# Two slots instead of four for an expert's token numbers and gates, three weight chunks split earlier, and semaphores raised earlier in a routed MLP

## The chip, the cores and the metric

The kernel runs on one core of one Trainium2 chip. The metric is the device time of one execution in microseconds (us). Three runs of the kernel before gave 426.74, 427.00 and 428.26 us, the median being 427.0. Engines are named TensorE (PE, its weight loads PEld), VectorE (DVE), ScalarE (ACT), GpSimd (POOL) and SyncE (SP).

## The reference

Three stages follow one another, all in float32.

```python
# linear attention with decay, B, H, S, D = 2, 8, 768, 48
for t in range(S):
    cur = einsum('bhd,bhe->bhde', u * k[t], v[t])
    y[t] = einsum('bhd,bhde->bhe', r[t], state + cur)
    state = w * state + einsum('bhd,bhe->bhde', k[t], v[t])
# MLP on x = y as 1536 rows of 384, 2048 wide
h = x @ w_in
x = (max(h, 0) + alpha * min(h, 0)) @ w_out
# routed MLP: 8 experts, 1024 wide, each row to its best expert, capacity 384
expert = argmax(x @ w_gate, axis=1);  gate = softmax(x @ w_gate)[expert]
disp[expert, place in order of rows] = x
out[row] = gate[row] * (max(disp[e] @ w1[e], 0) @ w2[e])[place]
```

## The kernel before

**Numbers.** Each float32 product is made of three matmuls of a faster type. A value is split into a high part (a ScalarE copy) and a low part (value less high part, a subtraction on VectorE or GpSimd), and high x high, high x low and low x high are added in PSUM. So every weight chunk, every activation and every routed row passes through a "high" and a "low" operation. split_high and split_low do this for the chunks, named by their number c; the eight chunks of an expert follow one another, and chunks 16 to 31 belong to experts 0 and 1.

**Stages.** Attention runs to about 65 us, the first MLP in four groups of 384 rows to about 270 us, and the routed MLP to the end. While the first MLP makes its rows, they are scattered by indirect DMAs to a table in HBM, a stretch for each expert. The first 256 rows of expert 0 are worked early. After that the experts follow in turn: expert 0 written out by itself, then experts 1 to 7. A block of 384 rows (three tiles of 128) is loaded for each expert, and the counts of rows are read into registers, which choose the path at run time. With up to 128 rows an expert takes the short path: flip_up multiplies the 128 rows with the whole first weight matrix in two halves of 512 columns (L1702), VectorE applies the relu (flip_relu, L1215), TensorE turns the result (flip_turn, L1723), ScalarE and VectorE make its high and low parts (flip_high, L848, and flip_low, L1221), and flip_down multiplies it with the second matrix (L1652, L1667). Between the two halves of flip_turn the rows of the next expert are turned (turn_xe, L1570) and split (xe_high, L817, and xe_low, L1175). With more than 128 rows it is expert_up for eight chunks (L1601), each followed by relu (ScalarE, L793) and relu_low (VectorE, L1159), then expert_down for the second tile (L1632) and flip_down for the first. A third tile is added above 256 rows. In this data experts 0, 5, 6 and 7 go the short way, experts 1 to 3 the one for two tiles, and expert 4 has three. (Expert 0's count is after the early rows are taken off.)

**Weights of experts 2 to 7.** SyncE loads w1 and w2 pieces into w1_raw and w2_raw. In the turn of expert e, ScalarE and VectorE split w2 of expert e+1 (split_high2, L810, and split_low2, L1166). When e's own rows are through the first matrix (s_w1free), ScalarE splits w1 of expert e+2 (split_high1, L801, in w1_and_y), and GpSimd makes the low parts (split_low1, L636). Among the copies of w1_and_y stand the y_copy (L834) of expert e, which scale its rows by their gates; GpSimd scatters them to the output by their token numbers (y_scatter, L612).

**Token numbers and gates.** A loaded row carries its token number and its gate behind its 384 values. keep_meta(e) on VectorE (a cast, L1183, and a copy, L1184) takes them out of the loaded block xe, of which there are two, into the buffers token and gate, of which there are four. It runs at the end of VectorE's turn for expert e-1. It may overwrite a slot only when the scatters that read it have landed. For that it waits for s_gone, which starts at 1 and which GpSimd raises in its own turn for expert e (1 to 6), behind the eight split_low1 of expert e+2 and a wait for the scatters up to expert e-1:

```python
                if 0 < e < E - 1:
                    pool.wait_ge(s_out, e * 16 * GT)
                    pool.sem_inc(s_gone, 1)
                for i in Y_ORDER:
                    y_scatter(e, i, s_out if e < E - 1 else s_last)
```

**Order.** Nothing plans this at run time: each engine's instructions are written out in order, and semaphores bind the engines together. All that stands behind a wait in an engine's queue waits too. Around expert 0, ScalarE has split_high(29) and (30), flip_high(0, 0, first half), xe_high(1, 0), split_high(31), flip_high(0, 0, second half), xe_high(1, 1) and (1, 2), then w1_and_y(0). VectorE has the two flip_relu, flip_low, xe_low(1, 0), flip_low, xe_low(1, 1) and (1, 2), split_low(29) to (31) for the second matrix, and keep_meta(1). GpSimd makes the low parts of these chunks' first matrix itself (L508). SyncE's load_xe(e) waits for s_meta, the count of keep_meta done, to reach e-1.

Of the kernel before, what the change touches and what calls it, by code (L numbers as in the profile page):

```python
# [3 lines left out]
P = 128  # L4


def attention_moe_kernel(nc, att_rk, att_v, decay, bonus, chunks, alpha, w_gate, out, disp,
# [8 lines left out]
    f32, f32r, bf16, i32 = mybir.dt.float32, mybir.dt.float32r, mybir.dt.bfloat16, mybir.dt.int32  # L16
# [15 lines left out]
    GT = G // P  # L32
# [115 lines left out]
    slot_i = mlp.take("slot_i", [P, GT], i32)  # L148
    xe = mlp.take("xe", [P, 2, GT, ROW], f32)
    y_out = mlp.take("y_out", [P, 2, GT, DM], f32)  # L150
    token = mlp.take("token", [P, 4, GT], i32)
    gate = mlp.take("gate", [P, 4, GT], f32)
    early_token = mlp.take("early_token", [P, ET], i32)
    early_gate = mlp.take("early_gate", [P, ET], f32)
    late = Region(phase_from, LIMIT)
# [13 lines left out]
    with ctx:  # L169
# [311 lines left out]
        def _(pool):  # L481
# [127 lines left out]
            def y_scatter(e, i, done=s_out):  # L609

                pool.wait_ge(s_yo, e * GT + Y_ORDER.index(i) + 1 + C_YO)
                pool.indirect_dma_start(  # L612
                    out=out, out_offset=bass.IndirectOffsetOnAxis(ap=token[:, e % 4, i:i + 1], axis=0),
                    in_=y_out[:, e % 2, i, :], in_offset=None, bounds_check=N - 1,
                    oob_is_err=False).then_inc(done, 16)

# [35 lines left out]
        def _(act):  # L652
# [167 lines left out]
            def y_copy(e, i):  # L820

                act.wait_ge(s_yzero, 1)
                act.wait_ge(s_meta, e + 1)
                act.wait_ge(s_gone, max(e - 1, 0) + C_GONE)
                if e == 1:
                    act.wait_ge(s_outa, 16 * ET)

                if i:
                    act.wait_ge(s_yd[i], e + 1)
                    if 0 < e < E - 1:  # L830
                        act.wait_ge(s_tel, e * GT + GT - i + 1)
                else:
                    act.wait_ge(s_step, e * NFE + NFE + FFN_STEPS)
                act.activation(y_out[:, e % 2, i, :], bank[4 + i][:, 0:DM], ACT.Copy,  # L834
                               scale=gate[:, e % 4, i:i + 1]).then_inc(s_yo, 1)

            act.wait_ge(s_cnti, 2)
            rows = [rows_of(act, e) for e in range(E)]
# [24 lines left out]
            with act.Else():  # L863
# [3 lines left out]
                    flip_high(0, i)  # L867
                for i in range(1, GT):
                    y_copy(0, i)
            for c in range(2 * NF - 3, 2 * NF - 1):  # L870
                split_high(c)
            flip_high(0, 0, (0,))
            xe_high(1, 0, bank[X_BANK[0]])
            split_high(2 * NF - 1)
            flip_high(0, 0, (1,))
            for i in range(1, GT):
                xe_high(1, i, bank[X_BANK[i]])
# [33 lines left out]
        def _(dve):  # L911
# [266 lines left out]
            def keep_meta(e):  # L1178

                xe_there(dve, e, range(GT))  # L1180

                dve.wait_ge(s_gone, max(e - 3, 0) + C_GONE)
                dve.tensor_copy(token[:, e % 4, :], xe[:, e % 2, :, DM:DM + 1].rearrange("p a b -> p (a b)"))  # L1183
                dve.tensor_copy(gate[:, e % 4, :], xe[:, e % 2, :, DM + 1:ROW].rearrange("p a b -> p (a b)"))\  # L1184
                   .then_inc(s_meta, 1)

            early_low(4)
# [44 lines left out]
            with dve.Else():  # L1232
                for i in range(1, GT):
                    xe_low(0, i, bank[8 - i])
                for i in range(1, GT):
                    for half in range(2):
                        flip_relu(0, i, half)
                    for half in range(2):
                        flip_low(0, i, half)
            flip_relu(0, 0, 0)  # L1240
            flip_relu(0, 0, 1)
            flip_low(0, 0, 0)
            xe_low(1, 0, bank[X_BANK[0]])
            flip_low(0, 0, 1)
            for i in range(1, GT):
                xe_low(1, i, bank[X_BANK[i]])
            for c in range(2 * NF - 3, 2 * NF):
                split_low(c)
            keep_meta(1)

            for e in range(1, E):
# [39 lines left out]
        def _(pe):  # L1291
# [387 lines left out]
            def no_tile(i):  # L1679

                pe.sem_inc(s_yd[i], 1)
# [84 lines left out]
            def expert(e, b):  # L1766

                rows = rows_of(pe, e)
                with pe.If(rows < P + 1):
                    pe.wait_ge(s_tel, (e - 1) * GT + GT)  # L1770
                    pe.sem_inc(s_mh, NFE)
                    for half in range(2):
                        flip_up(e, 0, half, b)
                    flip_turn(e, 0, (0,))
                    if more(e):
                        for i in range(GT):
                            x_bank_free(e, i)
                            turn_xe(e + 1, i, bank[X_BANK[i]], 1 - b)
                    no_tile(1)
                    flip_turn(e, 0, (1,))  # L1780
                with pe.Else():
                    pe.wait_ge(s_tel, (e - 1) * GT + GT)
                    pe.sem_inc(s_fh[0], 2)
                    pe.sem_inc(s_ft[0], 2)
                    expert_ups(e, 2 * P, b)
                    expert_down(e, 1, b)
                with pe.If(rows < 2 * P + 1):
                    flip_down_high(e, 0, 0, b)
                    pe.sem_inc(s_w1free, 1)
                    pe.sem_inc(s_fh[2], 2)  # L1790
                    no_tile(2)
                    flip_down_low(e, 0, 0, b)
                    flip_down_high(e, 0, 1, b)
                    flip_down_low(e, 0, 1, b)
                    pe.sem_inc(s_ft[2], 2)
                with pe.Else():
                    for half in range(2):
                        flip_up(e, 2, half, b)
                    pe.sem_inc(s_w1free, 1)
                    expert_down(e, 0, b, range(HF))  # L1800
                    flip_turn(e, 2)
                    expert_down(e, 0, b, range(HF, NFE))
                    flip_down(e, 2, b)
# [71 lines left out]
```

## Time and profile before

| | |
|---|---|
| median of three runs | 427.0 us (426.74 to 428.26) |
| the profiled execution | 427.0 us, span 425.3 us |
| TensorE matmul busy | 404.7 us, 95% |
| VectorE busy | 259.7 us, 61% |
| GpSimd busy | 230.7 us, 54% |
| ScalarE busy | 192.2 us, 45% |
| TensorE's share of the chain that ended last | 68% |
| granted TensorE clock, mean | 0.997 |

The span runs from the first instruction to the last, and the execution's own time is 1.7 us longer. TensorE is busy for nearly all of it; the others have slack on average, but each of them can be the last to be ready at a given point. In a timeline row the first number is the start from the span's beginning, the second the duration, and a bracket at the end says how long the engine had been idle before and for whom it waited. Operations of one engine overlap a little at their ends in these rows.

### The profile page before, as it was taken

What the parts mean: (1) busy time and instruction counts of PE and PEld (TensorE: products, weight loads), DVE (VectorE), ACT (ScalarE), POOL (GpSimd) and SP (SyncE); (2) the same over time, 40 slices, a digit from 0 to 9 for tenths busy, and PEclk for the clock granted to TensorE, in tenths of its full rate; (3) what the DMA queues carried; (4) which work ended last, traced back from release to release, by engine and by line L of the source; (5) the groups of instructions that cost most, each with busy time, mean ns of one, the idle gap of its engine ahead of it and who ended that gap; (6) DMA issues with size and microseconds to landing.
All of it is one profiled execution on the core that took longest, in us unless ns stands there. A gap on an engine that the chain in (4) does not pass through costs nothing.

```text
span 425.3 us, 9352 instructions
## 1 busy us (share of the span) xinstructions
PE 404.7 (95%) x3194; PEld 387.6 (91%) x3195; DVE 259.7 (61%) x523; ACT 192.2 (45%) x442; POOL 230.7 (54%) x239
## 2 busy tenths in 40 slices
PE   5799999999999999999999999999999999999893
PEld 4688899999999999999999999998998989899682
DVE  6888877765436344263343888573977594735960
ACT  2879955441311113111132243345849577536851
POOL 3999818563322633236353586054949375528862
PEclk9999999999999999999999999999999999999998
DMA  7997027437970100001000256039976685817500
GB/s 242 403 364 242 3 73 215 142 93 260 370 254 2 37 19 0 0 0 37 19 0 0 74 173 191 28 98 327 311 259 197 207 234 187 270 35 225 178 11 28
DMA packets 34330, 61.74 MB, mean 145 GB/s; under 512 B 4798, under 2 KB 27310, under 8 KB 34288
## 3 DMA queue, kind: packets, MB, share of 16 engines
q1 hardware_dynamic: 31280, 55.92, 40.3%
q0 software_dynamic: 3008, 5.29, 3.6%
q8 instruction: 22, 0.36, 0.4%
q14 instruction: 20, 0.16, 0.1%
HBM read 47.92 MB, written 15.18 MB: 148 GB/s over the span
## 4 chain that ended last, share of the span: by engine, by line
PE 68%; DVE 11%; issue 6%; ACT 5%; PEld 5%; POOL 2%; PEldq 1%; DMA 0%; ACTq 0%; DVEq 0%; POOLq 0%
PE bank L1418 24%; PE bank L1379 23%; DVE w_low L1166 4%; PE bank L1702 3%; PE bank L1363 3%; ACT w_high L801 3%; PE bank L1327 2%; PEld bank L1632 2%; PE bank L1355 2%; DVE expert_g_low L1159 2%; PE bank L1519 2%; PE bank L1632 2%; PE bank L1652 1%; PE bank L1313 1%; DVE xe_low L1175 1%
## 5 line engine op out<-in xcount | busy, mean ns | idle before, releaser
L554 POOL TENSOR_TENSOR g_low<-act_full,g_high 128x384 fp32r<-128x384 f32 x63 | 65.2, 1035 | 111.2 <-ACT g_high L708 111.1
L708 ACT ACTIVATE g_high<-act_full 128x384 fp32r<-128x384 f32 x64 | 33.7, 526 | 146.8 <-DVE act_full L1041 134.2
L1379 PE MATMUL bank<-x_split,w_high 128*128 (+1 forms) x384 | 98.6, 337 | 0.2 <-DVE w_low L954 0.2
L1035 DVE TENSOR_SCALAR neg<-bank,alpha_sb 128x384 f32<-128x384 f32 x64 | 39.4, 616 | 89.2 <-PE bank L1379 89.2
L636 POOL TENSOR_TENSOR w_low<-w_raw,w_high 128x384 fp32r<-128x384 f32 x48 | 52.9, 1137 | 33.9 <-ACT w_high L801 33.9
L1379 PEld LDWEIGHTS bank<-x_split,w_high 128*128 128x128 f32 x384 | 68.9, 188 | 0.9 <-DVE w_low L954 0.5
L1418 PE MATMUL bank<-w_high,g_high 128*128 128x384 f32 x189 | 64.5, 341 | 0.0
L1379 PE MATMUL bank<-x_split,w_low 128*128 (+1 forms) x192 | 64.4, 336 | 0.0
L1418 PE MATMUL bank<-w_high,g_low 128*128 128x384 f32 x189 | 63.8, 338 | 0.0
L1418 PE MATMUL bank<-w_low,g_high 128*128 128x384 f32 x189 | 63.8, 338 | 0.0
L1041 DVE SCALAR_TENSOR_TENSOR act_full<-bank,neg 128x384 f32<-128x384 f32 x64 | 35.7, 557 | 2.4
L1166 DVE TENSOR_TENSOR w_low<-w_raw,w_high 128x384 fp32r<-128x384 f32 x48 | 36.4, 775 | 0.3 <-ACT w_high L810 0.3
L1418 PEld LDWEIGHTS bank<-w_high,g_high 128*128 128x128 f32 x189 | 35.4, 187 | 0.8 <-POOL g_low L554 0.7
L1379 PEld LDWEIGHTS bank<-x_split,w_low 128*128 128x128 f32 x192 | 36.0, 188 | 0.0
L1418 PEld LDWEIGHTS bank<-w_low,g_high 128*128 128x128 f32 x189 | 35.5, 188 | 0.0
L1418 PEld LDWEIGHTS bank<-w_high,g_low 128*128 128x128 f32 x189 | 35.4, 187 | 0.0
L954 DVE TENSOR_TENSOR w_low<-w_raw,w_high 128x384 fp32r<-128x384 f32 x44 | 32.0, 755 | 0.0
L612 POOL DMA_INDIRECT out<-y_out,token x24 | 25.0, 1043 | 10.8 <-issue 5.4
L679 ACT ACTIVATE scores<-ident,diag 128x128 f32<-128x128 f32 x96 | 29.3, 394 | 2.6 <-DVE diag L969 2.6
L1601 PE MATMUL bank<-xe_high,w_high 128*128 128x256 f32 x96 | 27.7, 289 | 0.0
L662 ACT ACTIVATE w_high<-w_raw 128x768 fp32r<-128x768 f32 x32 | 26.8, 836 | 1.2 <-DMA w_raw<-chunks 1.2
L1601 PE MATMUL bank<-xe_high,w_low 128*128 128x256 f32 x96 | 27.1, 282 | 0.0
(171 smaller groups left out, 847.5 us busy)
## 6 DMA issues: line engine op xcount, KB each, us to landing
w_raw<-chunks SPq DMA_DIRECT2D x96, 192.0 KB, 4.4
w_raw<-chunks SPq DMA_DIRECT2D x32, 384.0 KB, 3.7
rk_in<-att_rk SPq DMA_DIRECT2D x12, 704.0 KB, 6.1
routed_rows<-fill SPq DMA_DIRECT2D x1, 5211.0 KB, 18.0
xe<-routed_rows SPq DMA_DIRECT2D x7, 579.0 KB, 4.4
v_in<-att_v SPq DMA_DIRECT2D x12, 200.0 KB, 5.7
out<-fill SPq DMA_DIRECT2D x1, 2304.0 KB, 23.3
x_split<-x_split POOLq DMA_DIRECT2D x18, 48.0 KB, 2.7
```

Source lines behind the costliest of these rows:

```text
L554: pool.tensor_tensor(gl[:, f % 4, :], act_full[:, f % 2, :], gh[:, f % 4, :].bitcast(f32), ALU.subtract).then_inc(s_gl, 1)
L636: pool.tensor_tensor(wl[:, slot, 0:W1], raw1[:, f, :], wh[:, slot, 0:W1].bitcast(f32), ALU.subtract).then_inc(s_wl1e, 1)
L662: act.activation(wh[:, slot, :], raw[:, m, :], ACT.Copy).then_inc(s_wh, 1)
L679: last = act.activation(scores[:, t % 2, h % 2, h // 2, :], ident[:, :], ACT.Copy, scale=diag[:, t % 2, h:h + 1])
L708: act.activation(gh[:, f % 4, :], act_full[:, f % 2, :], ACT.Copy).then_inc(s_gh, 1)
L954: dve.tensor_tensor(wl[:, slot, part], raw[:, m, part], wh[:, slot, part].bitcast(f32), ALU.subtract).then_inc(s_wl1 if first else s_wl2, 1)
L1035: dve.tensor_scalar(neg[:, f % 2, :], h, 0.0, alpha_sb[:, f:f + 1], ALU.min, ALU.mult)\
L1041: dve.scalar_tensor_tensor(act_full[:, f % 2, :], h, 0.0, neg[:, f % 2, :], ALU.max, ALU.add)\
L1166: dve.tensor_tensor(wl[:, slot, W1:CW], raw2[:, f, :], wh[:, slot, W1:CW].bitcast(f32), ALU.subtract).then_inc(s_wl2, 1)
L1379: last = mm(bank[f % 4][:, 0:G], a[:, f, w], x[:, kc, bass.ds(g * G, G)], start=kc == 0 and i == 0, stop=kc == KC - 1 and i == 2)
L1418: last = mm(bank[4 + i][:, 0:DM], a[:, f % 4, i * P:(i + 1) * P], w[:, slot, W1:CW], start=f == 0 and m == 0, stop=f == n - 1 and m == 2)
L1601: last = mm(bank[f % 4][:, 0:n], a[:, slot, w], x[:, b, kc, 0:n], start=kc == 0 and i == 0, stop=kc == KC - 1 and i == 2)
```

## The change

Four edits are made together.

- token and gate have two slots, indexed by e % 2. keep_meta(e) waits for s_gone to reach max(e-1, 0) + 1 instead of max(e-3, 0) + 1.
- ScalarE splits chunk 31 right behind chunks 29 and 30, ahead of flip_high(0, 0, (0,)) and xe_high(1, 0).
- VectorE makes the low parts of chunks 29 to 31 between flip_relu(0, 0, 0) and flip_relu(0, 0, 1), not behind xe_low(1, 2).
- TensorE, in an expert of at most 256 rows, raises s_w1free, s_fh[2] and s_yd[2] before flip_down instead of after its first eight matmuls, and on the short path s_yd[1] after the second half of flip_turn instead of before it.

```diff
-    token = mlp.take("token", [P, 4, GT], i32)
-    gate = mlp.take("gate", [P, 4, GT], f32)
+    token = mlp.take("token", [P, 2, GT], i32)
+    gate = mlp.take("gate", [P, 2, GT], f32)
...
# y_scatter (GpSimd) and y_copy (ScalarE): e % 4 becomes e % 2
...
# ScalarE
-            for c in range(2 * NF - 3, 2 * NF - 1):
+            for c in range(2 * NF - 3, 2 * NF):
                 split_high(c)
             flip_high(0, 0, (0,))
             xe_high(1, 0, bank[X_BANK[0]])
-            split_high(2 * NF - 1)
             flip_high(0, 0, (1,))
...
# VectorE, keep_meta(e)
-                dve.wait_ge(s_gone, max(e - 3, 0) + C_GONE)
-                dve.tensor_copy(token[:, e % 4, :], xe[:, e % 2, :, DM:DM + 1].rearrange("p a b -> p (a b)"))
-                dve.tensor_copy(gate[:, e % 4, :], xe[:, e % 2, :, DM + 1:ROW].rearrange("p a b -> p (a b)"))\
+                dve.wait_ge(s_gone, max(e - 1, 0) + C_GONE)
+                dve.tensor_copy(token[:, e % 2, :], xe[:, e % 2, :, DM:DM + 1].rearrange("p a b -> p (a b)"))
+                dve.tensor_copy(gate[:, e % 2, :], xe[:, e % 2, :, DM + 1:ROW].rearrange("p a b -> p (a b)"))\
                    .then_inc(s_meta, 1)
...
# VectorE, expert 0
             flip_relu(0, 0, 0)
+            for c in range(2 * NF - 3, 2 * NF):
+                split_low(c)
             flip_relu(0, 0, 1)
             flip_low(0, 0, 0)
             xe_low(1, 0, bank[X_BANK[0]])
             flip_low(0, 0, 1)
             for i in range(1, GT):
                 xe_low(1, i, bank[X_BANK[i]])
-            for c in range(2 * NF - 3, 2 * NF):
-                split_low(c)
             keep_meta(1)
...
# TensorE, expert(e, b)
+                    flip_turn(e, 0, (1,))
                     no_tile(1)
-                    flip_turn(e, 0, (1,))
...
                 with pe.If(rows < 2 * P + 1):
-                    flip_down_high(e, 0, 0, b)
                     pe.sem_inc(s_w1free, 1)
                     pe.sem_inc(s_fh[2], 2)
                     no_tile(2)
-                    flip_down_low(e, 0, 0, b)
-                    flip_down_high(e, 0, 1, b)
-                    flip_down_low(e, 0, 1, b)
+                    flip_down(e, 0, b)
                     pe.sem_inc(s_ft[2], 2)
```

## Rows read from the trace of the kernel before

**Rows 1.** Busy time by stretch: PE, PEld, DVE, ACT, POOL, clock, DMA share, GB/s

```profile
300.00:330.00 30.00, 28.82 (x216) 28.36 (x215) 24.13 (x44) 22.17 (x55) 23.21 (x21) 1.00 0.77 248
```

**Rows 2.** Waits from 290 us: engine line, releaser: us in total, times, longest

```profile
PE bank L1632 <- DVE xe_low L1175: 2.9, 4, 0.9
```

**Rows 3.** Timeline of TensorE, experts 0, 1, 2 and 6

```profile
295.67 0.60 PE L1723 MATMUL bank<-ident,expert_g_by_token 128*128 128x128 f32 x4
...
310.37 0.44 PE L1632 MATMUL bank<-w_high,expert_g_high 128*128 128x384 f32 x1 [0.32 <-DVE xe_low L1175]
...
329.42 0.44 PE L1632 MATMUL bank<-w_high,expert_g_high 128*128 128x384 f32 x1 [0.86 <-DVE xe_low L1175]
...
402.89 0.66 PE L1723 MATMUL bank<-ident,expert_g_by_token 128*128 128x128 f32 x4 [1.73 <-DVE expert_g_by_token L1215]
```

**Rows 4.** Timeline of GpSimd, experts 0, 1 and 5

```profile
292.39 2.00 POOL L508 TENSOR_TENSOR w_low<-w_raw,w_high 128x384 fp32r<-128x384 f32 x2
...
317.47 8.54 POOL L636 TENSOR_TENSOR w_low<-w_raw,w_high 128x384 fp32r<-128x384 f32 x8 [5.12 <-ACT w_high L801]
...
394.89 9.49 POOL L636 TENSOR_TENSOR w_low<-w_raw,w_high 128x384 fp32r<-128x384 f32 x8 [2.16 <-ACT w_high L801]
```

**Rows 5.** Line L646: whole run, from 335, from 394 us; ns min/median/max, starts

```profile
L646 POOLq EVENT_SEMAPHORE  x6: 17/17/17, 321.3 to 409.8; - x6
...
L646 POOLq EVENT_SEMAPHORE  x1: 17/17/17, 340.3 to 340.3; - x1
...
L646 POOLq EVENT_SEMAPHORE  x1: 17/17/17, 398.7 to 398.7; - x1
```

**Rows 6.** Timeline of VectorE, end of expert 1 and start of expert 2

```profile
317.73 0.80 DVE L1183 CAST token<-xe 128x3 int32<-128x3 f32 x1
...
322.00 0.42 DVE L1159 SCALAR_TENSOR_TENSOR expert_g_low<-bank,expert_g_high 128x256 fp32r<-128x256 f32 x1 [3.40 <-ACT expert_g_high L793]
```

**Rows 7.** Lines L1183 (whole run) and L1166 (expert 2): ns min/median/max

```profile
L1183 DVE CAST token<-xe x8: 154/792/989, 289.9 to 408.4; 128x3 int32<-128x3 f32 x8
...
L1166 DVE TENSOR_TENSOR w_low<-w_raw,w_high x8: 542/544/1418, 322.4 to 331.3; 128x384 fp32r<-128x384 f32 x8
```

**Rows 8.** Timeline of VectorE, end of expert 5 and start of expert 6

```profile
397.62 0.99 DVE L1183 CAST token<-xe 128x3 int32<-128x3 f32 x1
...
398.60 0.68 DVE L1215 TENSOR_SCALAR expert_g_by_token<-bank 128x512 f32<-128x512 f32 x1
399.55 2.68 DVE L1166 TENSOR_TENSOR w_low<-w_raw,w_high 128x384 fp32r<-128x384 f32 x2 [0.28 <-ACT w_high L810]
402.16 0.68 DVE L1215 TENSOR_SCALAR expert_g_by_token<-bank 128x512 f32<-128x512 f32 x1
```

**Rows 9.** Timeline of VectorE, expert 0

```profile
292.40 0.69 DVE L1215 TENSOR_SCALAR expert_g_by_token<-bank 128x512 f32<-128x512 f32 x1 [2.30 <-PE bank L1702]
294.45 0.69 DVE L1215 TENSOR_SCALAR expert_g_by_token<-bank 128x512 f32<-128x512 f32 x1 [1.36 <-PE bank L1702]
...
298.81 3.66 DVE L954 TENSOR_TENSOR w_low<-w_raw,w_high 128x384 fp32r<-128x384 f32 x3
...
303.36 0.41 DVE L1159 SCALAR_TENSOR_TENSOR expert_g_low<-bank,expert_g_high 128x256 fp32r<-128x256 f32 x1
```

**Rows 10.** Line L388, chunks 30 and 31: issues, and us to landing

```profile
L388 SPq DMA_DIRECT2D w_raw<-chunks x2: 375/398/421, 287.2 to 287.8; - x2
...
DMA to landing us min/median/max: 5.1/5.9/6.7
```

**Rows 11.** Timeline of ScalarE, expert 0 and start of expert 1

```profile
292.32 0.85 ACT L662 ACTIVATE w_high<-w_raw 128x768 fp32r<-128x768 f32 x1 [0.98 <-DMA w_raw<-chunks]
...
295.83 0.85 ACT L662 ACTIVATE w_high<-w_raw 128x768 fp32r<-128x768 f32 x1
...
301.57 0.41 ACT L793 ACTIVATE expert_g_high<-bank 128x256 fp32r<-128x256 f32 x1
```

**Rows 12.** Line L1795, TensorE's queue: ns min/median/max, starts

```profile
L1795 PEldq EVENT_SEMAPHORE  x6: 51/51/51, 315.7 to 415.1; - x6
```

More of the change, by code:

```diff
@@ L612, in y_scatter @@
                 pool.indirect_dma_start(
-                    out=out, out_offset=bass.IndirectOffsetOnAxis(ap=token[:, e % 4, i:i + 1], axis=0),
+                    out=out, out_offset=bass.IndirectOffsetOnAxis(ap=token[:, e % 2, i:i + 1], axis=0),
                     in_=y_out[:, e % 2, i, :], in_offset=None, bounds_check=N - 1,
@@ L834, in y_copy @@
                 act.activation(y_out[:, e % 2, i, :], bank[4 + i][:, 0:DM], ACT.Copy,
-                               scale=gate[:, e % 4, i:i + 1]).then_inc(s_yo, 1)
+                               scale=gate[:, e % 2, i:i + 1]).then_inc(s_yo, 1)
             act.wait_ge(s_cnti, 2)
```

## The prediction

> **What bounds the kernel now.** I read the busy time by stretch first. TensorE is busy for 28.8 of the 30 us from 300 to 330, with the clock fully granted, while VectorE has 24.1 and GpSimd 23.2 [rows 1]. So the routed part, where every edit lies, is bound by TensorE with little idle, and an edit counts only by what it does to the few places where TensorE waits. The waits list says where these are: expert_down (L1632) waited 2.9 us in 4 times for xe_low on VectorE [rows 2]. The TensorE timeline gives them singly: 0.32 us in expert 1, 0.86 in expert 2, and 1.73 before the second gate-transposition (L1723) of expert 6 [rows 3]. Experts 1 to 4 take the path for over 128 rows, experts 0, 5, 6 and 7 the short one with flip_turn. Matmuls between the waits are packed, and whatever a wait adds is paid in full. VectorE, ScalarE and GpSimd run in chains that begin anew with each expert from TensorE's semaphores, so a delay of TensorE moves what follows and is not made up there.
>
> The profiled execution took 427.0 us, its span being 425.3 with 1.7 outside; the median of the three runs is 427.0 too, so changes of the span are added to 427.0 directly. About 0.5%, 2.1 us, is what a measurement of this kernel can tell from no change.
>
> **Part 1: keep_meta waits for two experts later.** token and gate go from four slots to two. That frees some SBUF and removes no instruction. The wait in keep_meta(e+1), on VectorE in expert e's turn, rises from s_gone at least e-1 to at least e+1. The (e+1)th count is added by GpSimd in its own iteration e (L646), behind the eight split_low1 of expert e+2 and a wait for the scatters of expert e-1. Behind the waiting VectorE stand relu_low(e+1, 0) (L1159) or flip_relu (L1215), and for these TensorE waits.
>
> When does the count come? GpSimd works at the eight subtractions from 317.47 to 326.01 [rows 4], but the increment at L646 stands in the trace at 321.3, in the next expert at 340.3 and in expert 5 at 398.7 [rows 5]. GpSimd's queue has thus handed over all eight when ScalarE has written the last w_high, and counts while the engine still works. So VectorE waits for ScalarE's last split_high1, not for GpSimd's work.
>
> In expert 1 keep_meta stands at 317.73 and the next relu_low at 322.00, which waited 3.40 us for ScalarE [rows 6]. Now the cast starts at about 321.35. Beside a busy GpSimd a cast takes 0.79 (the median of eight, 0.15 the least, 0.99 the most [rows 7]), and the next operation begins 0.8 to 0.98 after its start. That gives relu_low at 322.15 to 322.33, later by 0.15 to 0.33. In experts 1 to 3 that lands on the chain of VectorE which ends in TensorE's waits of some 0.86. I take 0.2, three times: **0.6 us** (0 to 1.0).
>
> Expert 4: the count comes late, since its w1_and_y waits for the third tile's y, but VectorE then has nothing before flip_relu(5), whose first half is needed by TensorE only after the second half of flip_up. I take nothing, at most 0.4. Expert 6: L646's last event is at 409.8 [rows 5], before flip_relu(7) would be due; nothing, at most 0.5.
>
> Expert 5 is dearer. keep_meta(6) starts at 397.62 and flip_relu(6, 0, 0) at 398.60, the subtractions (L1166) at 399.55, the second flip_relu follows, and TensorE waits for that one for 1.73 [rows 3, 8]. Now the cast starts at 398.75, flip_relu at 399.73 (+0.98), it ends at 400.35, and the subtractions begin 0.8 later than 399.55. All of it is in front of TensorE's wait: **0.8 us** (0.3 to 1.4, because the two subtractions, 2.68 us for both, run in turns with GpSimd's and may lose or win part of a turn).
>
> **Part 2: the last three chunks of expert 1 before flip_relu(0, 0, 1).** On ScalarE split_high(31) moves ahead of flip_high(0, 0, 0) and xe_high(1, 0); on VectorE three split_low (L954) move from behind xe_low(1, 2) to between the two flip_relu of expert 0. No instruction is added. Today the two flip_relu are at 292.40 and 294.45, and the three subtractions take 3.66 us from 298.81 [rows 9]. TensorE takes the second half's transposition at 295.67 without a wait [rows 3]. What sets the new time is chunk 31. The two load_chunk issues are at 287.2 and 287.8, and their landings take 5.1 and 6.7 us [rows 10]; as ScalarE stopped waiting for chunk 30 at 292.32 [rows 11], the 6.7 belongs to chunk 31: landed at 294.5. ScalarE copies it in 0.85 [rows 11], ready 295.3. VectorE has done the other two by then (from 293.09; GpSimd is at its own two until 294.39 [rows 4]). The third subtraction starts at 295.3, as does GpSimd's for the same chunk. One takes 0.54 us alone and up to 1.42 beside GpSimd [rows 7]; the three today average 1.22. I take 1.2 since both are released by one semaphore. So flip_relu(0, 0, 1) starts at 296.4, and TensorE 0.73 later (402.16 to 402.89 in expert 6 [rows 3, 8]), at 297.1 instead of 295.67: +1.4, between +0.8 (VectorE first) and +1.8.
>
> The Trainium skill, page "SBUF — State Buffer", on the ports of VectorE and GpSimd, says that a VectorE operation with two SBUF inputs and a GpSimd operation that reads SBUF take a shared port as an exclusive lock, the second being blocked until the first ends. By it the third subtraction has one of the two ends and not the mean; its order of issue decides, and the sum would be 0.6 us lower or 0.2 higher. The rows of 0.54 and 1.42 agree [rows 7].
>
> What comes back: VectorE is free of 3.66 us before expert 1. relu_low(1, 0) stands at 303.36 behind the subtractions and keep_meta(1), though ScalarE's relu was there at 301.57 [rows 9, 11]. With TensorE 1.4 later, relu(1, 0) ends about 303.3, so VectorE's chain stays where it is in time, and TensorE's wait of 0.32 at 310.37 is gone. ScalarE is 0.8 later with split_high1(2), which is still less than TensorE's delay. Net **1.1 us** (0.5 to 1.5). SP's order is untouched; its load_xe waits for s_meta, but behind load_w1 for GpSimd's work, which is later still.
>
> **Part 3: TensorE's own semaphores.** s_w1free, s_fh[2] and s_yd[2] are raised earlier by the eight matmuls of flip_down_high(e, 0, 0), and no_tile(1) after four transpositions instead of before. For experts 1 to 3 ScalarE's w1_and_y is held by flip_high(e, 2), which waits for s_ft[2] at L1795 (first event 315.7 [rows 12]), and that stays last. In experts 5 and 6 ScalarE comes to split_high1 later than w1free in any case. VectorE's flip_relu(e, 2), whose result nobody uses when the expert has no third tile, may start a little earlier and then waits for ScalarE as before. The order of matmuls is the same. Nothing, 0 to -0.3.
>
> **The sum:** 0.6 + 0.8 + 1.1 = 2.5 us, 427.0 + 2.5 = **429.5 us**. If this is right, the worst stall is still that before L1723 of expert 6, 2.5 us then.
>
> **Rivals.** (a) *The shifts are mostly absorbed.* The third subtraction goes first at the port (+0.5 net), the casts cost 0.14 each (0.4), and expert 5 wins part of a turn (0.3 to 0.4): 1.3 us, 428.3. The spread of the casts and of the subtractions speaks for it; against it, that before a busy GpSimd the long times are the common ones.
>
> (b) *Not slower: chunk 31 lands early.* It decides at L954: if the chunk lands in the 5.1 us of its neighbour, at 292.9, ScalarE has it by 294.0 and VectorE does three subtractions in a row from 293.09, ending near 295.2. TensorE then loses 0.1 to 0.5 and gets back 0.32 in expert 1. It holds up to a landing at about 293.5. With 0.4 to 0.8 of part 1 the time is 427.5. The transfers of eight w1 pieces are issued right behind and share the DMA engines, which speaks for 6.7 again.
>
> (c) *GpSimd counts only when its work is done.* Then keep_meta(2) would go at 326.0 [rows 4] and relu_low(2, 0) be 4.2 late; without GpSimd beside it VectorE wins back about 1.9 on three subtractions, leaving 2.3, three times 6.9. Expert 4 adds 1, expert 5 waits until 404.4 (394.89 and 9.49 [rows 4]) and costs 4 at the second flip_relu. With part 2, 13 us: 440. The events of L646 speak plainly against it.
>
> (d) *The port turns go worse*: 1.8 in part 2, 1.4 in expert 5, 0.33 per cast, 0.9 in experts 4 and 6: 5 us, 432.
>
> **How the numbers follow.** The forecast 0.46, (a) 0.25, (b) 0.12, (c) 0.07, (d) 0.10. The forecast's own span is 428.8 to 430.6. The range 427.4 to 432.6 holds all but (c) and the ends of the others. Slower by over 0.5% (above 429.1): five sixths of the forecast, (c) and (d), 0.56. Faster by over 0.5% (below 424.9) has no case that I can name: 0.02. The rest, 0.42, is within.
>
> **What would show it.** In the new profile: the cast of keep_meta at 321 to 323 and not 318, right behind L646's event, and relu_low(2, 0) 0.8 to 1.0 after it; no gap at L1632 of expert 1; a new gap of about 1.4 us before the second L1723 of expert 0; a gap of about 2.5 before that of expert 6; L646's events still some 4 us ahead of the end of GpSimd's eighth subtraction. It is wrong if the cast begins only when GpSimd is through, if TensorE has no gap in expert 0, or if a stall stands where I found none, in experts 4 and 6.

## The result

The changed kernel takes 430.78 us (median of 8 runs, 429.95 to 433.21) where the kernel before takes 427.04 (8 runs). The ratio is 1.0089 with a 95% interval of 1.0062 to 1.0115: 3.8 us slower (2.6 to 4.9), of which 2.5 had been forecast. The profiled execution, at 429.56 us and a span of 427.9, is the fastest of them, 2.6 us above that of before.

The profile of the changed kernel, busy time over the whole span (the kernel before has the same 9352 instructions):

```profile
span 427.9 us, 9352 instructions
PE 406.9 (95%) x3194; PEld 388.8 (91%) x3195; DVE 258.3 (60%) x523; ACT 192.6 (45%) x442; POOL 229.8 (54%) x239
```

The counts of instructions are the same for every engine. What moved is found in the timeline of TensorE, whose waits answer to [rows 3]. Of its rows with a gap, one of each kind is shown:

```profile
296.25 0.66 PE L1722 MATMUL bank<-ident,expert_g_by_token 128*128 128x128 f32 x4 [0.83 <-DVE expert_g_by_token L1214]
...
323.82 0.38 PE L1600 MATMUL bank<-xe_high,w_high 128*128 128x256 f32 x1 [0.18 <-DVE expert_g_low L1158]
329.88 0.44 PE L1631 MATMUL bank<-w_high,expert_g_high 128*128 128x384 f32 x1 [0.55 <-DVE xe_low L1174]
...
401.88 0.63 PE L1722 MATMUL bank<-ident,expert_g_by_token 128*128 128x128 f32 x4 [0.46 <-DVE expert_g_by_token L1214]
404.28 0.66 PE L1722 MATMUL bank<-ident,expert_g_by_token 128*128 128x128 f32 x4 [0.79 <-DVE expert_g_by_token L1214]
405.56 0.44 PE L1651 MATMUL bank<-w_high,expert_g_high 128*128 128x384 f32 x1 [0.62 <-DVE w_low L1165]
...
416.10 0.41 PE L1651 MATMUL bank<-w_high,expert_g_high 128*128 128x384 f32 x1 [0.53 <-issue]
```

There are four kinds of new gap: one before expert 0's second transposition (L1722), one in the middle of the first-matrix products of experts 2 to 4 (L1600), one before the first transposition of expert 6 (0.46), and one before the first matmul of flip_down (L1651) in experts 6 and 7. The old gap at L1631 of expert 1 is gone. The old wait of 1.73 before the second transposition of expert 6, which the prediction saw grow to 2.5, is 0.79. A list of gaps does not yet give what each edit cost, because a delay can hide in a later wait. For that I took each landmark's start less the start of flip_up of expert 0 in the same execution, and subtracted the same of the kernel before. The table gives this difference, the lag, in us, for the changed kernel and for the three edits made alone (below):

| landmark in TensorE's order | changed | slots alone | early split alone | semaphores alone |
|---|---|---|---|---|
| expert 0, second flip_turn | 0.99 | 0.00 | 1.88 | 0.00 |
| expert 1, expert_down | 0.46 | 0.00 | 1.35 | 0.21 |
| expert 2, expert_down | 0.87 | 0.44 | 1.34 | 0.18 |
| expert 3, expert_down | 1.34 | 0.91 | 2.31 | 0.23 |
| expert 4, expert_down | 1.82 | 1.36 | 2.31 | 0.27 |
| expert 5, second flip_turn | 1.81 | 1.36 | 2.29 | 0.25 |
| expert 5, flip_down | 2.24 | 1.36 | 2.29 | 0.69 |
| expert 6, second flip_turn | 1.80 | 1.64 | 2.52 | 0.29 |
| expert 6, flip_down | 2.43 | 1.64 | 2.52 | 0.92 |
| expert 7, flip_down | 2.99 | 1.65 | 4.04 | 1.45 |

(The changed kernel came to flip_up 0.41 us early, so that its span shows 2.6 and not 3.0.)

The end of VectorE's turn for expert 1 in the changed kernel, which answers to [rows 6]:

```profile
321.40 1.07 DVE L1182 CAST token<-xe 128x3 int32<-128x3 f32 x1 [3.56 <-POOLq L646]
322.39 1.06 DVE L1183 COPY gate<-xe 128x3 f32<-128x3 f32 x1
323.36 0.41 DVE L1158 SCALAR_TENSOR_TENSOR expert_g_low<-bank,expert_g_high 128x256 fp32r<-128x256 f32 x1
```

And GpSimd's work and its count at L646, which answer to [rows 4, 5]:

```profile
317.50 8.18 POOL L636 TENSOR_TENSOR w_low<-w_raw,w_high 128x384 fp32r<-128x384 f32 x8 [5.66 <-ACT w_high L801]
...
L646 POOLq EVENT_SEMAPHORE  x6: 17/17/17, 321.3 to 411.2; - x6
```

The cast starts 0.1 us after the count at 321.3, while GpSimd works until 325.7. So the count does run ahead of the engine. But the cast is held for 1.07 us and then the copy for 1.06 as well, where the copy had never cost more than 0.16 before. Each takes as long as one GpSimd subtraction (1.0) and ends with it.

### The profile page after: what moved, and what is told of

It reads as the page before. It is cut to its first block, busy times and chain, and to the rows that moved or that the text cites. A ratio compares the mean times of both kernels' runs of the same rounds, so it can differ in the third digit from the quotient of the medians.

```text
span 427.9 us, 9352 instructions
## 1 busy us (share of the span) xinstructions
PE 406.9 (95%) x3194; PEld 388.8 (91%) x3195; DVE 258.3 (60%) x523; ACT 192.6 (45%) x442; POOL 229.8 (54%) x239
## 4 chain that ended last, share of the span: by engine, by line
PE 69%; DVE 9%; issue 5%; PEld 5%; POOL 4%; DMA 3%; ACT 2%; SPq 0%; PEldq 0%; POOLq 0%; ACTq 0%; DVEq 0%
PE bank L1417 24%; PE bank L1378 23%; POOL w_low L636 4%; PE bank L1362 3%; PE bank L1701 3%; DVE w_low L1165 3%; PE bank L1326 3%; PE bank L1354 2%; PE bank L1651 2%; PE bank L1631 2%; PEld bank L1600 2%; PEld bank L1631 2%; DMA w_raw<-chunks 2%; PE bank L1312 1%; DVE expert_g_low L1158 1%
## 5 line engine op out<-in xcount | busy, mean ns | idle before, releaser
L636 POOL TENSOR_TENSOR w_low<-w_raw,w_high 128x384 fp32r<-128x384 f32 x48 | 50.8, 1090 | 37.8 <-ACT w_high L801 37.8
L1165 DVE TENSOR_TENSOR w_low<-w_raw,w_high 128x384 fp32r<-128x384 f32 x48 | 33.5, 714 | 0.0
L612 POOL DMA_INDIRECT out<-y_out,token x24 | 25.9, 1079 | 12.0 <-issue 5.5
L953 DVE TENSOR_TENSOR w_low<-w_raw,w_high 128x384 fp32r<-128x384 f32 x44 | 31.2, 736 | 0.2 <-ACT w_high L662 0.2
L1600 PE MATMUL bank<-xe_high,w_high 128*128 128x256 f32 x96 | 28.1, 293 | 0.7 <-DVE expert_g_low L1158 0.5
L1600 PE MATMUL bank<-xe_high,w_low 128*128 128x256 f32 x96 | 27.1, 282 | 0.0
```

Of the source, the lines that this page charges most:

```text
L636: pool.tensor_tensor(wl[:, slot, 0:W1], raw1[:, f, :], wh[:, slot, 0:W1].bitcast(f32), ALU.subtract).then_inc(s_wl1e, 1)
L953: dve.tensor_tensor(wl[:, slot, part], raw[:, m, part], wh[:, slot, part].bitcast(f32), ALU.subtract).then_inc(s_wl1 if first else s_wl2, 1)
L1165: dve.tensor_tensor(wl[:, slot, W1:CW], raw2[:, f, :], wh[:, slot, W1:CW].bitcast(f32), ALU.subtract).then_inc(s_wl2, 1)
L1600: last = mm(bank[f % 4][:, 0:n], a[:, slot, w], x[:, b, kc, 0:n], start=kc == 0 and i == 0, stop=kc == KC - 1 and i == 2)
```

## Each edit alone

All times below are against runs of the kernel before on the same chip. Its median went from 427.2 to 428.5 between these chips, so the ratios count, not the medians.

**The slots alone.** The kernel before with two slots (token and gate as [P, 2, GT], indexed by e % 2) and the wait of the change:

```diff
+                dve.wait_ge(s_gone, max(e - 1, 0) + C_GONE)
```

> The kernel before with two slots and the stronger wait of keep_meta alone. Theory 1 (from the changed kernel's trace): in experts 1 to 3 the cast starts 3.5 us later, with ScalarE's last split_high1, and then both small operations of keep_meta (1.07 and 1.06 us) wait for a GpSimd subtraction each; the first L1632 of experts 2, 3, 4 moves by 0.43 to 0.48 more each time, and in expert 5 the delay is made up again: span +1.3 us, time about 428.4. Theory 2 (the prediction's sizes): 0.2 each in experts 1 to 3 and 0.8 in expert 5, +1.4, so the same time but with the stall before the second L1723 of expert 6 longer than 2.3 us. Theory 3: the wait is nothing, 427.0.

Measured: 428.48 us, ratio 1.0023 (1.0009 to 1.0037), +1.0 us. Its trace has keep_meta as in the changed kernel:

```profile
321.17 1.07 DVE L1183 CAST token<-xe 128x3 int32<-128x3 f32 x1 [3.57 <-POOLq L646]
322.15 1.06 DVE L1184 COPY gate<-xe 128x3 f32<-128x3 f32 x1
323.12 0.41 DVE L1159 SCALAR_TENSOR_TENSOR expert_g_low<-bank,expert_g_high 128x256 fp32r<-128x256 f32 x1
```

The lag grows by 0.44, 0.47 and 0.45 in experts 1 to 3 and by 0.28 in expert 5. Theory 1 holds for the place, though in expert 5 the delay is not made up in full; the stall of over 2.3 us in expert 6 that theory 2 wanted isn't there.

**The early split alone.** ScalarE's and VectorE's part of the change's diff.

> The kernel before with chunks 29 to 31 split earlier on ScalarE and VectorE alone. Theory 1 (from the changed kernel's trace): about 1.0 us lost before the second transposition of expert 0, 0.55 won back in expert 1's first-matrix products and at its L1632: +0.45 us, about 427.5. Theory 2 (the prediction): +1.4 and 0.3 back, +1.1, 428.1. Theory 3: nothing is won back, because the wait of expert 1 comes from something else than VectorE's three subtractions: +1.0 with a wait of 0.3 still at L1632 of expert 1.

Measured: 428.23 us, ratio 1.0025 (1.0007 to 1.0043), +1.1 us. Its profiled execution, at 431.09 us, is the slowest of the twelve, so the trace shows where time can go and not what the edit costs as a rule. ScalarE's copies of chunks 30 and 31 in it, to be set against [rows 11]:

```profile
294.21 0.85 ACT L662 ACTIVATE w_high<-w_raw 128x768 fp32r<-128x768 f32 x1 [2.85 <-DMA w_raw<-chunks]
295.22 0.84 ACT L662 ACTIVATE w_high<-w_raw 128x768 fp32r<-128x768 f32 x1 [0.16 <-DMA w_raw<-chunks]
```

Chunk 31 was ready for its copy 5.1 us after flip_up's start at 290.09, against 4.5 in the changed kernel. Its transfer took as long in both (6.8 and 6.7 us), but was issued 0.6 later against flip_up. Chunk 30 was ready at 4.1 against 2.3, so that VectorE's second subtraction too had to wait. The third subtraction took 0.83 us, against 0.56. The second flip_turn of expert 0 was 1.88 late, in the changed kernel 0.99. Half a microsecond comes back both times in expert 1 (1.88 to 1.35, 0.99 to 0.46). So the price is set by when chunk 31 is there, and then by the turn of the third subtraction; both differ from one execution to the next. Two later jumps in this trace have nothing to do with the edit. The one in expert 3 is a single subtraction:

```profile
342.81 3.38 DVE L1165 TENSOR_TENSOR w_low<-w_raw,w_high 128x384 fp32r<-128x384 f32 x1
```

It ended only after three GpSimd operations in a row, and put TensorE back by 1.7 us, of which 0.8 were made up. The other, 1.6 us in flip_down of expert 6, is the clock. Busy time of PE, PEld, DVE, ACT and POOL, then the granted clock:

```profile
404.00:406.00 2.00, 0.56 (x4) 0.42 (x4) 2.00 (x4) 0.19 (x1) 2.00 (x3) 1.00 0.00 0
406.00:408.00 2.00, 2.00 (x7) 1.92 (x7) 2.00 (x5) 1.78 (x5) 1.85 (x2) 0.57 0.00 0
408.00:410.00 2.00, 2.00 (x8) 2.00 (x8) 2.00 (x6) 2.00 (x5) 1.39 (x3) 0.58 0.02 0
```

**The semaphores alone.** TensorE's part of the change's diff.

> The kernel before with only TensorE's semaphore increments moved. Theory 1 (from the changed kernel's trace): where TensorE's queue has run empty at the second flip_turn, the increments now stand between it and the first weight load of flip_down, so L1651 starts 0.3 to 0.6 us later in experts 5, 6 and 7: +1.2 to +1.5 us, about 428.4, a gap marked before the first matmul of flip_down in experts 6 and 7. Theory 2 (the prediction): 0 to -0.3 us, no such gap; then the gap in the changed kernel comes from its other edits.

Measured: 428.25 us, ratio 1.0022 (1.0008 to 1.0036), +0.9 us. TensorE in experts 6 and 7:

```profile
404.44 0.43 PE L1652 MATMUL bank<-w_high,expert_g_high 128*128 128x384 f32 x1 [0.62 <-DVE w_low L1166]
...
414.95 0.41 PE L1652 MATMUL bank<-w_high,expert_g_high 128*128 128x384 f32 x1 [0.53 <-issue]
```

The first gap names a releaser, w_low, that had long been done; the second, of the same kind, says "issue". The lag grows by 0.63 in expert 6 and 0.53 in expert 7; the 0.44 of expert 5 is nearly made up at the wait in expert 6. The prediction's "nothing, 0 to -0.3" is refuted.

**Six more increments.** To see whether it is the increments themselves:

```diff
                     no_tile(2)
+                    for _ in range(6):
+                        pe.sem_inc(s_spare, 1)
                     flip_down(e, 0, b)
```

> As the kernel before with the moved increments, and six further increments of a semaphore nobody reads behind the moved ones, ahead of flip_down. Theory 1: each increment costs TensorE's queue a fixed time where it has run empty, so the gap before the first matmul of flip_down grows in experts 5, 6 and 7 by six times that, some 0.3 to 0.9 us in each, and experts 1 to 3, where matmuls are queued ahead, show nothing: 429 to 431. Theory 2 (the gap has another cause): the time of the kernel with the moved increments, within 0.3 us.

Measured: 431.70 us, ratio 1.0104 (1.0075 to 1.0133), +4.4 us. TensorE, the six increments in its queue in expert 5, and busy times and clock in expert 7:

```profile
392.20 0.44 PE L1653 MATMUL bank<-w_high,expert_g_high 128*128 128x384 f32 x1 [1.14 <-issue]
...
404.91 0.43 PE L1653 MATMUL bank<-w_high,expert_g_high 128*128 128x384 f32 x1 [1.54 <-ACT expert_g_high L849]
...
416.40 0.58 PE L1653 MATMUL bank<-w_high,expert_g_high 128*128 128x384 f32 x1 [1.50 <-ACT y_out L835]
...
L1793 PEldq EVENT_SEMAPHORE  x6: 51/51/51, 391.0 to 391.8; - x6
...
416.00:418.00 2.00, 1.60 (x5) 1.63 (x6) 0.41 (x1) 0.77 (x2) 0.90 (x1) 0.62 0.06 16
418.00:420.00 2.00, 2.00 (x8) 2.00 (x8) 0.00 (x0) 0.00 (x0) 1.04 (x2) 0.53 0.06 9
```

Six increments stretch from 391.0 to 391.8, some 0.15 us apart although each is shown with 0.051. The gaps grew by 0.95, 0.92 and 0.97 over those with the moved increments alone, 0.16 for each. On the short path four increments were moved to stand ahead of flip_down: s_yd[1], s_w1free, s_fh[2] and s_yd[2]. At 0.16 each they are 0.64, and the lag of the run above grew by 0.63 in expert 6 and by 0.53 in expert 7. Experts 1 to 3 show nothing; that matmuls are queued ahead there is the likely reason. Not all of the 4.4 us is the increments': in this trace what expert 5 lost is made up in expert 6, and 1.5 us are lost in flip_down of expert 7, where the granted clock (third figure from the end) fell to 0.62 and 0.53.

## Undoing each edit

**Three slots.** `token` and `gate` with e % 3 and `max(e - 2, 0)` in the changed kernel.

> The changed kernel with three slots for token and gate, keep_meta(e) waiting for s_gone at least max(e-2, 0) + 1 and so for GpSimd's iteration before this one. Theory 1: that count is there an expert earlier, keep_meta costs nothing again, the casts start right behind flip_low, and 1.0 to 1.4 us of the change's 2.6 go: span about 426.7. Theory 2 (the prediction): some 1.4 us go as well, of which 0.8 before the second L1723 of expert 6. Theory 3 (the loss is in the other two edits): no difference to the changed kernel.

Measured: 430.26 us, ratio 1.0065 (1.0040 to 1.0091). The casts are back in their place and the gaps at L1631 back at 0.83 to 0.84 with no gap at L1600. By the table's measure it gains 1.1 over the changed kernel at the last flip_down (1.90 against 2.99), although expert 0 was held for 0.3 longer, its third subtraction having taken 0.85 us and not 0.56. The sizes agree with theory 1; the intervals of the timed runs overlap.

**Early split undone.**

> The changed kernel with the split of chunks 29 to 31 back in its old place on ScalarE and VectorE. Theory 1: 0.4 to 0.5 us go, and the wait of 0.3 at L1632 of expert 1 comes back. Theory 2 (the prediction): 1.1 us go. A third: the loss in expert 0 is merely moved to a later wait, no difference.

Measured: 429.58 us, ratio 1.0049 (1.0030 to 1.0068), 1.7 us less than the changed kernel's ratio gives, and 0.4 in the profiled execution (2.61 against 2.99). The wait before expert 1's expert_down is back:

```profile
310.42 0.44 PE L1632 MATMUL bank<-w_high,expert_g_high 128*128 128x384 f32 x1 [0.37 <-DVE xe_low L1175]
```

In the changed kernel's profiled execution chunk 31 landed 4.5 us after the start of flip_up; in the other traces that show it, it was 4.2 to 5.3. Over the timed runs the edit costs more than that execution shows, though the two intervals overlap.

**Semaphores undone.**

> The changed kernel with TensorE's increments back in their old places. Theory 1: the gaps of 0.62 and 0.53 before flip_down's first matmul in experts 6 and 7 go, and what expert 5 lost (0.36), part of which is hidden by VectorE's chain before the second L1723 of expert 6: 1.1 to 1.3 us less than the changed kernel. Theory 2 (the prediction): no difference, or 0.3 more.

Measured: 429.38 us, ratio 1.0050 (1.0032 to 1.0068), 1.7 us less than the changed kernel's ratio gives, the two intervals just overlapping; the first matmul of flip_down follows the transposition without a gap in experts 5 to 7. Expert 6 waits longer for VectorE in it (lag 2.63 at the second flip_turn, against 1.80), so in the profiled execution only 0.4 of the gain is left (2.63 against 2.99). What took the rest is keep_meta in expert 5, whose copy waited a full turn here and not in the changed kernel (0.15):

```profile
400.88 1.04 DVE L1183 COPY gate<-xe 128x3 f32<-128x3 f32 x1
```

Without these 0.89 us the gain would be 1.25, by estimate, within theory 1's 1.1 to 1.3.

## What stands in TensorE's way: five more kernels

**The subtractions put off.** The waits at L1632 in the kernel before were the largest in sum [rows 2]. The edit, on the path for over 128 rows:

```diff
-                        if FIRST <= e + 1 < E:
-                            split_low2(e + 1, f)
+                        if FIRST <= e + 1 < E and f >= 4:
+                            split_low2(e + 1, f - 4)
+                    if FIRST <= e + 1 < E:
+                        for f in range(4, NFE):
+                            split_low2(e + 1, f)
```

> The kernel before, with VectorE's split_low2(e+1, f) on the path for more than 128 rows put off by four chunks, so that the first four relu_low follow each other while GpSimd is at its subtractions. If TensorE's wait of 0.86 us at L1632 in experts 2 to 4 (0.32 in expert 1) comes from VectorE's subtractions run in turns with GpSimd's, it goes: 2 to 2.9 us less, 424.3 to 425. If it comes from ScalarE's late relu, nothing changes: 427.0.

Measured: 423.49 us, ratio 0.9905 (0.9878 to 0.9932), -4.1 us. The profiled execution is 1 us above the median: in expert 6 it lost 1.6 us of its gain again to the clock (0.64 and 0.51 in 400 to 404 us). TensorE's waits from 290 us, and VectorE in expert 2:

```profile
PE bank L1726 <- DVE expert_g_by_token L1215: 2.1, 2, 1.8
...
321.27 0.43 DVE L1159 SCALAR_TENSOR_TENSOR expert_g_low<-bank,expert_g_high 128x256 fp32r<-128x256 f32 x1 [3.41 <-ACT expert_g_high L793]
321.95 0.42 DVE L1159 SCALAR_TENSOR_TENSOR expert_g_low<-bank,expert_g_high 128x256 fp32r<-128x256 f32 x1 [0.26 <-ACT expert_g_high L793]
...
328.86 2.42 DVE L1166 TENSOR_TENSOR w_low<-w_raw,w_high 128x384 fp32r<-128x384 f32 x5
```

No wait at L1632 is left: the lag is -0.59, -1.71, -2.80 and -3.89 at the four expert_down. The five subtractions behind take 2.42 together, 0.48 each, now that GpSimd is through, where the first ones had taken 1.04 and 1.42 beside it. The gain is 0.59 in expert 1 and 1.1 in each of experts 2 to 4, more than the gaps of 0.32 and 0.86 of [rows 3]. The weight loads at the same two moments had waited just that long, in the kernel before:

```profile
310.37 0.19 PEld L1632 LDWEIGHTS bank<-w_high,expert_g_high 128*128 128x128 f32 x1 [0.56 <-issue]
...
329.42 0.19 PEld L1632 LDWEIGHTS bank<-w_high,expert_g_high 128*128 128x128 f32 x1 [1.09 <-DVE w_low L1166]
```

**Only chunks 29 and 30 early.** Chunk 31 stays where it was, on ScalarE and VectorE.

> The kernel before, with only the low parts of chunks 29 and 30 moved between the two flip_relu of expert 0 on VectorE; chunk 31 keeps its old place on ScalarE and comes behind xe_low(1, 2) on VectorE. Theory 1 (what the early split costs is the landing of chunk 31, which VectorE has to wait for in the full edit): the second L1723 of expert 0 is 0.2 to 0.6 us late, more only if chunk 30 lands late as well, and 0.56 comes back in expert 1: 426.7 to 427.2. Theory 2 (the cost is VectorE's time for the subtractions themselves): two thirds of the full edit's 1.0, 427.8.

Measured: 427.73 us, ratio 0.9987 (0.9969 to 1.0006), which can't be told from no change. The second flip_turn of expert 0 is not late (lag -0.02) and the 0.58 comes back in expert 1. VectorE between the two flip_relu:

```profile
292.76 0.85 DVE L954 TENSOR_TENSOR w_low<-w_raw,w_high 128x384 fp32r<-128x384 f32 x1
293.90 0.56 DVE L954 TENSOR_TENSOR w_low<-w_raw,w_high 128x384 fp32r<-128x384 f32 x1 [0.29 <-ACT w_high L662]
294.38 0.68 DVE L1215 TENSOR_SCALAR expert_g_by_token<-bank 128x512 f32<-128x512 f32 x1
```

Two subtractions fit in the time that VectorE had to wait for TensorE anyway. So it was chunk 31 with the third subtraction behind it, and not the time of the other two. As in the early split alone, one subtraction of expert 3 took 3.37 us and the clock fell in expert 6, so that the profiled execution ends with a lag of 2.1. How often the timed ones did is open; the gain of 0.58 is shown by the trace alone.

**Two slots with a late keep_meta.** keep_meta(e) in expert e's own turn, behind its last relu_low or xe_low:

```diff
+                    if e > 1:
+                        keep_meta(e)
...
-                if e < E - 1:
-                    keep_meta(e + 1)
```

> The kernel before with two slots, keep_meta(e) for e of 2 and more moved into expert e's own turn: behind the eighth relu_low on the path for more than 128 rows, behind the last xe_low on the short path. By then GpSimd's iteration e-1 has long counted, and in experts 2 to 4 its subtractions are over. Theory 1 (the change's cost is the place of keep_meta in front of the next expert's first operation, beside GpSimd): the 1.3 us of the two-slot kernel go, 427.2 or, as the first operations of experts 2 to 4 are no longer behind it at all, a little less; at most 1 us may be lost in expert 6, as load_xe(7) and the w2 pieces behind it are issued some 4 us later. Theory 2 (the two slots themselves hold something up, a scatter or a scaled copy): it stays at 428.5.

Measured: 426.64 us, ratio 0.9962 (0.9945 to 0.9979). Nothing of the slots' 1.0 us is left, and the lag stays at 0.0 until expert 5 and ends at -0.58, for the wait in expert 6 fell from 1.73 to 1.29:

```profile
403.25 0.66 PE L1725 MATMUL bank<-ident,expert_g_by_token 128*128 128x128 f32 x4 [1.29 <-DVE expert_g_by_token L1215]
```

Two slots cost nothing; the place of keep_meta did.

**All subtractions late, on the short path too.**

> Two slots with the late keep_meta, split_low2 put off by four chunks on the long path, and on the short path all eight split_low2 behind the last xe_low, so that no subtraction beside GpSimd stands in front of TensorE. Expected: the 3.7 us of the kernel with the put-off subtractions alone, and 1.7 more from the wait before the second L1723 of expert 6, if VectorE's two subtractions there are its cause, with a steadier clock there: 421.5 to 422.5. If the w2 subtractions, now last in their turn, come too late for flip_down of the next short expert, the gain of 1.7 turns up as a wait at L1652 instead: 423.5.

Measured: 426.10 us, ratio 0.9937 (0.9916 to 0.9959), 1.4 us more than the put-off alone by the ratios, though the intervals overlap. Neither expectation was right. The wait in expert 6 grew:

```profile
398.94 0.63 PE L1726 MATMUL bank<-ident,expert_g_by_token 128*128 128x128 f32 x4 [3.23 <-DVE expert_g_by_token L1215]
...
390.61 7.49 DVE L1166 TENSOR_TENSOR w_low<-w_raw,w_high 128x384 fp32r<-128x384 f32 x7
398.02 1.28 DVE L1215 TENSOR_SCALAR expert_g_by_token<-bank 128x512 f32<-128x512 f32 x2
...
400.00:404.00 4.00, 4.00 (x19) 4.00 (x17) 2.54 (x5) 2.75 (x8) 3.23 (x4) 0.57 0.02 1
```

On the long path the put-off subtractions came to lie behind GpSimd's work; on the short path they came to lie beside it, seven of them at 1.07 each, and the next expert's flip_relu stood behind them. After TensorE's wait the clock was down for a stretch of 4 us.

**The two that worked, together.** The put-off on the long path, and two slots with the late keep_meta:

> Two slots with the late keep_meta, and split_low2 put off by four chunks on the long path only; the short path's subtractions stay where they are. The put-off is worth about 3.9 us of TensorE's waits in experts 1 to 4, the late keep_meta 0.5 in expert 6: about 1.0% less than the kernel before, 423 us where that takes 427. If the short path's late subtractions were not what cost the earlier combined kernel its 2.7 us in expert 6, it will stay near 426.

Measured: 422.49 us (422.46 to 422.64), ratio 0.9880 (0.9861 to 0.9900), 5.1 us less than the kernel before with half its slots: the lowest ratio of all, from four runs, with an interval that overlaps that of the put-off alone.

## Why the prediction was right, and where it was wrong

**Direction and total.** Slower by 2.5 was forecast, 3.8 measured (2.6 to 4.9): the direction is right, and 430.8 lies in the range, but just outside the forecast's own span of 428.8 to 430.6. The edits alone sum to 1.0 + 1.1 + 0.9 = 3.0. That the sum came so near is in part luck. By the table, the changed kernel lost 0.46 in expert 0 and 1 (forecast 1.1), 1.36 in the next three (0.6), won 0.44 on the way to expert 6's second flip_turn (forecast: lost 0.8), and lost 0.43, 0.63 and 0.56 to the increments (forecast: nothing). Errors of both signs made up 3.0.

**Part 1, when the count comes**: right. The event at L646 gave the moment to 0.1 us, and rival (c), which would have cost ten more, was rightly given a small chance.

**Part 1, sizes**: 0.6 in experts 1 to 3 and 0.8 in expert 5; with the slots alone it was 1.36 and 0.28. The step that failed is "the next operation begins 0.8 to 0.98 after its start". It counted one turn at the port for the cast and the old 0.15 for the copy. In all old rows the copy had slipped in right behind the cast; now, in experts 1 to 3, it waited a full turn (1.06, and relu_low began 1.96 after the cast). In expert 5 it did not in this trace, and did in that of the semaphores undone. What decides that was not found. In expert 5 VectorE made its delay up. flip_relu began 1.0 us later than TensorE's own lag accounts for. But from there to the next flip_relu it took 2.59 us instead of 3.56, because the two subtractions between took 2.07, not 2.68, and no longer waited 0.28 for ScalarE [rows 8]:

```profile
400.96 0.68 DVE L1214 TENSOR_SCALAR expert_g_by_token<-bank 128x512 f32<-128x512 f32 x1
401.56 2.07 DVE L1165 TENSOR_TENSOR w_low<-w_raw,w_high 128x384 fp32r<-128x384 f32 x2
403.55 0.68 DVE L1214 TENSOR_SCALAR expert_g_by_token<-bank 128x512 f32<-128x512 f32 x1
```

So the sign that the prediction named, a worst stall of 2.5 us before the second L1723 of expert 6, did not come: there are 0.46 and 0.79 there, and the worst stall is the 0.83 of expert 0. Nor does all that a wait adds stay lost, as the prediction had it. Here VectorE made a delay up in shorter turns, and TensorE made up the 0.44 of expert 5 at its next wait for VectorE.

**Part 2**: 1.1 forecast, 1.1 timed (0.3 to 1.8), 0.46 in the changed kernel's profiled execution. Its working was right in the mechanism (the landing of chunk 31 sets it) and mis-sized in two terms. The third subtraction, put at 1.2, went first at the port and took 0.56 us:

```profile
294.15 0.85 ACT L662 ACTIVATE w_high<-w_raw 128x768 fp32r<-128x768 f32 x1 [1.36 <-DMA w_raw<-chunks]
...
295.03 0.56 DVE L953 TENSOR_TENSOR w_low<-w_raw,w_high 128x384 fp32r<-128x384 f32 x1 [0.15 <-ACT w_high L662]
...
295.08 1.37 POOL L508 TENSOR_TENSOR w_low<-w_raw,w_high 128x384 fp32r<-128x384 f32 x1 [1.09 <-ACT w_high L662]
```

The Trainium skill, page "SBUF — State Buffer", section "SBUF: two separate sides", says that of two such operations the one that starts first gets the shared pair of ports for the whole instruction, while the other is blocked. The trace agrees: GpSimd's subtraction for the same chunk began 0.05 us later and took 1.37 us, where one by itself takes 1.0. But the prediction's "one of the two ends" is too narrow. In two other traces the third subtraction came while GpSimd was still at chunk 30's, waited out the rest of it, and took 0.83 and 0.85. (The prediction's upper end, too, is given once as 0.4 above its figure and once as 0.2; the 1.42 of its row gives 0.2.)

And 0.56 came back in expert 1, not 0.32: the wait of the weight load, and not the bracket of the matmul, is what there was to win.

**Part 3** is the step that was wrong: "Nothing, 0 to -0.3", measured +0.9 (0.3 to 1.5). I followed who is released by the increments, and not what they stand in front of. In experts 6 and 7 TensorE has just waited at the second flip_turn, so that no matmul is left in its queue to cover what follows; then each increment ahead of the next weight load is on the path, 0.16 us each.

**The rest.** Against the profiled execution the median is 1.2 us higher. Traces of single edits show two things that could make it up, a subtraction that takes 3.4 us (1.7, half of it made up) and the clock in expert 6 (1.6). The clock is on record for every timed execution. Two of the changed kernel's eight, at 433.0 and 433.2 us, have a mean of 0.992 and 0.993, the others 0.995 or more at 430.0 to 431.1. So the clock can account for these two and not for the median. What does is open.

## What to carry to other kernels

A semaphore increment costs its engine's queue time too: before moving one "earlier", see whether the engine's queue is empty there. Tiny VectorE copies from SBUF can cost a whole GpSimd operation each while GpSimd works (1.07 and 1.06 us here, 0.15 without it), so a wait that moves them beside it can cost by their count and not their size. And where two engines take turns, the work to put off is what nobody waits for, to where the other engine is idle; the same edit in a place where it isn't made things worse.

## What the runs showed of the hardware

- GpSimd's queue raised a semaphore at 321.3 us while its engine had over four of eight operations still to do (until 325.7).
- Increments in TensorE's queue follow each other at 0.15 to 0.16 us.
- In four traces the granted clock went from 1.00 (2.4 GHz) to averages of 0.50 to 0.64 over some 4 us of expert 6, its half level being 1.2 GHz. Before it TensorE had waited 1.75, 1.76, 1.78 and 3.23 us at the second flip_turn. It cost 1.6 us in three of them and 1.0 in the fourth. In the kernel before, after 1.73 us, and with the semaphores undone, after 1.74 and 0.85, it stayed at 1.00. With six more increments it fell in expert 7, after gaps of 0.35 and 1.50, and cost 1.5. The Trainium skill, page "TensorE: Matmul & The Clock Gate", section "What's actually happening", says that the chip's windows of observation run free of the kernel, so that the point of a change differs between runs; that fits, and no run here tests it.
- The mean clock of an execution goes with this: 0.990 to 0.993 in the five traces with a fall, 0.994 to 0.997 in the nine without. By that sign the clock fell in 24 of 83 timed executions of the kernel before too, and in 10 of 12 of the kernel with all subtractions late.
- One VectorE subtraction beside GpSimd took 3.4 us, through three GpSimd operations in a row, in two traces at the same place of expert 3. That is not rare as such: in every trace, that of the kernel before included, three subtractions of the first MLP at 249 to 258 us take 3.0, 2.3 and 3.2 us beside GpSimd.
